# Two lanes in one load: keys by token and values, the source read as lane, token, row

## The reference

```python
scores = scale * np.matmul(q, k.transpose(0, 1, 3, 2))
gamma = 1.0 - 2.0 ** (-5.0 - np.arange(H, dtype=np.float32))
Dmat = np.where(rel >= 0, gamma[:, None, None] ** rel[None, :, :], 0.0)
attn = np.matmul(scores * Dmat[None], v)
x = attn.transpose(0, 2, 1, 3).reshape(B * S, H * D)          # 2304 x 512
xn = x / rms * rms_g
y = (silu(xn @ w_gate) * (xn @ w_val)) @ w_out                # 512 -> 1536 -> 512
g = where(h >= 1, h, where(h <= -1, 0, (h + 1) ** 2 / 4))     # h = y @ w_in, 512 -> 2048
out = g @ w_out2                                              # 2048 -> 512
```

## Time and profile before

| | |
|---|---|
| median of 3 runs | 922.66 us (922.09 to 923.28) |
| profiled execution | 925.14 us, its span 923.4 us |
| PE busy | 873.4 us, 95% |
| PEld busy | 829.0 us, 90% |
| DVE busy | 479.3 us, 52% |
| ACT busy | 434.7 us, 47% |
| POOL busy | 261.9 us, 28% |
| DMA | 124.26 MB, mean 135 GB/s |
| granted TensorE clock, mean | 0.985 |

### The profile page before, as it was taken

One profiled execution on the slowest core, in us unless ns is written; L12 is line 12 of the kernel. 1 busy time (PEld: TensorE's weight loads), 2 busy tenths in 40 slices (PEclk: granted clock), 3 DMA queues, 4 the chain that ended last, 5 costly groups with the idle time before them and its releaser, 6 DMA issues.

```text
span 923.4 us, 18183 instructions
## 1 busy us (share of the span) xinstructions
PE 873.4 (95%) x7712; PEld 829.0 (90%) x7712; DVE 479.3 (52%) x646; ACT 434.7 (47%) x704; POOL 261.9 (28%) x179
## 2 busy tenths in 40 slices
PE   4767799999999999999999998999999999999998
PEld 4666799999999999999999998999999888888886
DVE  3587975577875553522341668765656632222220
ACT  2545654445754554432131457877779732222110
POOL 0224764444954666000040321403134200000000
PEclk9897999999999999999999999999999999999999
DMA  6777133223234534533543134243439664433340
GB/s 202 218 219 229 37 111 97 98 97 98 93 103 147 183 98 150 184 104 103 182 147 128 53 129 149 103 136 116 141 117 299 211 166 129 114 114 114 114 119 29
DMA packets 124096, 124.26 MB, mean 135 GB/s; under 512 B 6256, under 2 KB 93424, under 8 KB 124016
## 3 DMA queue, kind: packets, MB, share of 16 engines
q1 hardware_dynamic: 124016, 123.11, 42.1%
HBM read 80.62 MB, written 42.47 MB: 133 GB/s over the span
## 4 chain that ended last, share of the span: by engine, by line
PE 78%; DVE 6%; DMA 5%; SPq 5%; ACT 3%; issue 2%; POOL 1%; DVEq 0%; ACTq 0%
PE pair L640 13%; PE pair L642 13%; PE pair L641 13%; PE pair L775 7%; PE pair L774 7%; PE pair L773 7%; PE pair L739 6%; PE pair L740 6%; PE pair L741 6%; DMA a_kt<-ktok 1%; DVE cb L1343 1%; SPq L346 1%; SPq L349 1%; DMA b_scratch<-cb 1%; ACT cl L911 1%
## 5 line engine op out<-in xcount | busy, mean ns | idle before, releaser
L640 PE MATMUL pair<-xc,wc 128*128 128x288 f32 x672 | 199.6, 297 | 0.9 <-ACT cp L898 0.6
L641 PE MATMUL pair<-xc,wc 128*128 128x288 f32 x672 | 198.3, 295 | 0.0
L642 PE MATMUL pair<-xc,wc 128*128 128x288 f32 x672 | 197.7, 294 | 0.0
L898 ACT ACTIVATE cp<-pair 128x576 f32<-128x576 f32 x160 | 103.3, 647 | 153.0 <-PE pair L642 146.7
L1431 POOL TENSOR_TENSOR wc<-wt,wc 128x512 fp32r<-128x512 f32 x84 | 123.0, 1488 | 94.6 <-ACT wc L831 67.9
L640 PE MATMUL pair<-xc,wr 128*128 128x288 f32 x448 | 133.9, 299 | 6.9 <-ACT cp L898 6.3
L641 PE MATMUL pair<-xc,wr 128*128 128x288 f32 x448 | 132.3, 295 | 0.0
L642 PE MATMUL pair<-xc,wr 128*128 128x288 f32 x448 | 131.8, 294 | 0.0
L640 PEld LDWEIGHTS pair<-xc,wc 128*128 128x128 f32 x672 | 126.0, 187 | 1.8 <-issue 1.5
L642 PEld LDWEIGHTS pair<-xc,wc 128*128 128x128 f32 x672 | 126.6, 188 | 0.0
L641 PEld LDWEIGHTS pair<-xc,wc 128*128 128x128 f32 x672 | 126.2, 188 | 0.0
(11 more groups left out here) (95 smaller groups left out, 1452.3 us busy)
## 6 DMA issues: line engine op xcount, KB each, us to landing
b_scratch<-cb SPq DMA_DIRECT2D x32, 576.0 KB, 2.9
bv_r<-b_scratch SPq DMA_DIRECT2D x18, 1024.0 KB, 5.8
a_scratch<-cb SPq DMA_DIRECT2D x24, 576.0 KB, 2.9
av_r<-a_scratch SPq DMA_DIRECT2D x8, 1728.0 KB, 8.5
wt<-wB SPq DMA_DIRECT2D x72, 128.0 KB, 2.9
a_k<-kT SPq DMA_DIRECT2D x16, 288.0 KB, 4.1
a_q<-qT SPq DMA_DIRECT2D x16, 288.0 KB, 4.6
y_scratch<-yo SPq DMA_DIRECT2D x8, 576.0 KB, 3.7
```

What stands on the lines that cost most here:

```text
L640: pe.matmul(o, wh, xh, start=FIRST[i] and j == 0, stop=False, skip_group_check=True)
L641: pe.matmul(o, wh, xl, start=False, stop=False, skip_group_check=True)
L642: mm = pe.matmul(o, wl, xh, start=False, stop=j == 1, skip_group_check=True)
L898: act.activation(copied(g, n)[:, :, :], pair[(X, Q, X, X)[n]][:, :, 0:HALF], ACT.Copy).then_inc(s_c, 1)
```

## The change

The two loads of the keys by token, one a lane, become one load that writes all 128 rows, and so do the two loads of the first four chunks of the values. The source is read as lane, token, row: first the 64 tokens of lane 0, each 512 floats, then the 64 tokens of lane 1. The ninth chunk of the values keeps its load. The waits count one load of a_kt and two of a_v a unit.

```diff
-                for l in range(2):
-                    rows, some = slice(C * l, C * l + C), slice(NL * l, NL * l + NL)
-                    sp.dma_start(a_kt[rows, i, :, :], ktok[b, p, :, some, :]).then_inc(d_kt[i], 16)
-                for l in range(2):
-                    rows, some = slice(C * l, C * l + C), slice(NL * l, NL * l + NL)
-                    sp.dma_start(a_v[rows, p, 0:NL, :], vtok[b, p, :, some, :]).then_inc(d_v[p], 16)
+                def lanes(src):
+                    return src.rearrange("t (l j) d -> l t (j d)", l=2)
+
+                sp.dma_start(a_kt[:, i, :, :].rearrange("s j d -> s (j d)"), lanes(ktok[b, p])).then_inc(d_kt[i], 16)
+                sp.dma_start(a_v[:, p, 0:NL, :].rearrange("s j d -> s (j d)"),
+                             lanes(vtok[b, p, :, 0:2 * NL, :])).then_inc(d_v[p], 16)
                 sp.dma_start(a_v[0:C, p, NL, :], vtok[b, p, :, NC - 1, :]).then_inc(d_v[p], 16)
@@ states
-                pe.wait_ge(d_v[p], 48 * (b + 1))
+                pe.wait_ge(d_v[p], 32 * (b + 1))
@@ decayed
-                act.wait_ge(d_kt[i], 32 * (u // NK + 1))
+                act.wait_ge(d_kt[i], 16 * (u // NK + 1))
```

## The result

The changed kernel takes 1034.6 us (median of 3 runs, 1033.78 to 1035.08), the kernel before 922.66 us: 1.121 times as long, 95% interval 1.119 to 1.124. Its profiled execution took 1035.08 us with a span of 1033.3, against 925.14 and 923.4: 109.9 us more.

The account below looks back on a forecast made before the run. Load issuing and moving were both taken as near their limits in the attention stage. Two engines needing 205.0 us for sixteen units start later stages 112.5 us later: 925.1 + 112.5 = 1037.6, put at 1035 us for timed runs; range 1005 to 1110.

Parts of the forecast that it names:

- Two engines: Attention stage: merged loads, divided along a source outermost axis of 2, run on two DMA engines; slower, chance 0.87.
- The rate: Attention stage: engines 0 and 1 each carry 301,056 bytes a unit at 23.5 GB/s, 12.8 us a unit, 205.0 us for sixteen.
- one rival: Attention stage: two engines at the stage's mean rate, 16.6 to 17.5 us a unit, 1096 to 1110 us; chance 0.17.
- The weight loads: Attention stage: eight weight loads of 128 KB, 64 KB an engine at 17.7 GB/s, add 3.7 us.
- Do the two engines run dry?: Attention stage: they stay fed, as three key buffers leave two whole units, 25 us of work, queued.
- The last values: End of the attention stage: last values land at 211.6 us, with completion about 212 us.
- From the last values to the first product: Attention stage's end: the last unit's states, copy and outputs, with gaps, take 4.7 us; L640 may start at 216.7.
- The 1.3 us given back: First products: POOL has its share of the first weight unit done, so a pause goes, 1 to 1.5 us.
- The signs: Profile: DMA share 0.15 to 0.2, 85 to 100 GB/s, L791 every 12 to 13 us, load waits over 100 us.
- TensorE's clock: Attention stage: TensorE may run at its lower clock level, hidden there; 1 or 2 us at the first product.
- Spread over all engines: Attention stage: merged loads as wide as any other, two issues a unit saved, about 915 us, between 906 and 923; chance 0.10.
- nothing won: Attention stage: loads use all engines, but the 1.2 us saved a unit turns into a longer hold, 923 us; chance 0.03.

Follow-up runs that it names:

- the four runs with 2 to 16 groups: Changed kernel, keys and values stored by the host so the merged loads' outermost source axis counts 2, 4, 8 or 16: 1034.2, 953.9, 926.6, 925.4 us.
- plain rows: Changed kernel, host storing each unit's keys and first eight value chunks as 128 back-to-back rows of 2 KB: 917.8 us, 0.992 to 0.996 times before.
- gaps: Changed kernel, merged loads reading 128 rows of 2 KB with 512 bytes unused behind each row: 918.3 us, 0.993 to 0.997 times before.
- three axes: Changed kernel, merged loads reading 16 blocks of 8 rows of 2 KB, 512 bytes unused behind each block: 925.4 us, 1.000 to 1.004 times before.

## Why the prediction was right

The forecast was 1035 us and the measured 1034.6. Part of this closeness is chance, as the steps show.

*Two engines.* Right, and it was the choice on which the sign hung. The trace of before could not show it. The packets (960 fewer, and two in flight at once for more than half of the stage), the share of 0.13 with 51 GB/s, and the four runs with 2 to 16 groups do.

*The rate.* Taken as 23.5 GB/s from one microsecond with all engines busy, 12.8 us a unit. Measured: 24.6 over a whole unit, 12.25 us; 25.5 in a stretch with almost only merged loads. So sixteen units were put 16 x 0.56 = 9 us too long. The means of 17 to 18 GB/s, which one rival rested on, belong to a stage in which all sixteen engines work; two engines left to themselves were faster, and that rival falls. The upper bound of 26.5 was nearer to such an engine than the stage's mean.

*The weight loads.* Expected 3.7 us in line on the same two engines; the step that holds them took 15.60 against 12.25, so 3.35 us.

*Do the two engines run dry?* No, as forecast, but not for the reason given. I let the three buffers of keys set how far the queue runs ahead, by two units or 25 us. The keys of the fourth unit were free to be issued from 19 us on, when the first unit's were decayed, and were issued at 34.21, as the queue was held behind the loads of the third unit until then; its lead is the 15 us seen above, and that was enough.

*The last values.* Expected to be there at 212 us. L559 of the last unit starts at 204.93 us: 7 us earlier, where the rate alone gives 9; the other 2 weren't traced.

*From the last values to the first product.* Sized too small. I took 4.7 us, as the sum of the last unit's own steps. The end of the stage after, which answers to the earlier trace rows:

```profile
204.93 1.13 PE L559 MATMUL pair<-a_v,a_kd 64*64 64x64 f32 x32 [6.93 <-issue]
...
206.12 0.22 ACT L798 ACTIVATE a_S<-pair 128x64 f32<-128x64 f32 x1 [3.49 <-PE pair L559]
206.44 2.18 DVE L1136 SCALAR_TENSOR_TENSOR a_S<-a_S,cdec_s,pair 128x64 f32<-128x64 f32 x7 [7.51 <-ACT a_S L798]
...
206.83 1.94 PE L583 MATMUL pair<-a_q,a_S 64*64 64x64 f32 x31
...
208.81 0.60 ACT L803 ACTIVATE xr<-pair 128x512 f32<-128x512 f32 x1 [2.46 <-PE pair L583]
...
209.66 0.92 PE L576 MATMUL pair<-a_r,a_v 64*64 64x64 f32 x36 [0.89 <-ACT xr L805]
...
210.37 1.10 PE L583 MATMUL pair<-a_q,a_S 64*64 64x64 f32 x32
...
211.40 0.40 PE L640 MATMUL pair<-xc,wc 128*128 128x288 f32 x1
```

The code has `states(15)`, `outputs(14)`, `outputs(15)` in a row. So the outputs of the unit before (1.94) and their way out of PSUM (0.60 and the small copy) stand before the last unit's own, and the stretch takes 6.5 us. The earlier trace rows could have said so: the same two instructions, L559 and the first L640, are 6.23 us apart there (96.64 to 102.87).

*The 1.3 us given back* at the first products didn't come: from the first L640 to the first copy L898 it was 5.84 us before and is 5.90 now. POOL's parts of the first weights are queued between the outputs' decays of units 14 and 15, so it does them in the last microseconds as before, however long it idled earlier.

Together: 7 us too late at the last values, 1.8 and 1.3 us too short behind them. The first product was forecast at 216.7 and came at 211.40; with the give-back that didn't come the shift is 108.5 us, not 112.5. Another 1.3 us appeared in the long rest (816.0 us from the first copy to the end, 814.7 before), whose cause wasn't looked for. The profiled execution is 109.9 us longer, the medians of the runs 111.9; the forecast of 112.5 came nearer to the latter than its working deserves.

*The signs.* Three of those named came true: 98 GB/s over the stage, a start of L791 every 11.7 to 12.8 us but for the step with the weights, and the rest of the kernel as before but shifted. The share is 0.30 and not 0.15 to 0.2: I had counted the fourteen other engines as almost idle, yet each carries 38 KB a unit at the slower pace of all sixteen. ScalarE's wait for keys is 85.3 us and not over 100. How long a merged load takes to land the trace doesn't give; the keys of the fourth unit reached ScalarE 15 us after their issue, most of it in line.

*TensorE's clock.* As supposed, it fell: a granted clock of 0.50, the level of 1.2 GHz, from 108 to 116 us with TensorE busy for 0.56 us of the eight, and 0.70 over the stage. It was hidden: L559 takes 317 ns where it took 265, in a stage that waits for loads.

*The rivals.* "Spread over all engines" has its price tested in three runs: 917.8 with plain rows, 918.3 with gaps, 925.4 with three axes, against a forecast of about 915 with 906 and 923 as its bounds; the third lies above them. (The bytes of a unit in it were added up wrongly: 288 + 288 + 512 + 32 are 1120 KB, 1.147 MB, not 1088; at 248 GB/s that is 4.6 us and not 4.5. The two engines' share of 256 + 38 KB was right, so the forecast doesn't hang on it.) The bound of the queue alone was out of reach, since the queue turned to waiting for TensorE. The rival "nothing won" had named just this, a hold in place of the issues, and in part it is what happened; "spread and faster" had named VectorE and POOL as late next, and not TensorE.

## What to carry to other kernels

Before two transfers are merged, write down the axes of both sides as the transfer will carry them and look at the outermost one: here a count of 2 put 256 KB on two engines of sixteen and cost 112 us of 923, where the same bytes with 128 rows outermost, laid out so by the host, save 5 us. The count of small packets, one for each load and engine, tells in one line how wide the loads of a kernel really are. And a saved issue is worth only what lies between it and the next wait: 19 us of queue time became 5, since the queue soon stood waiting for a buffer that TensorE held.

## What the runs showed of the hardware

Three things that I had not expected. Two DMA engines left almost to themselves move rows of 2 KB at 25.5 GB/s each (51 GB/s together), while in the stage of before, with all sixteen at work and packets of all sizes, a busy engine averages 18.1. It is not only the mix: by the packet records a packet of 2 KB takes 112 ns on average there and 89 in the changed kernel, with a median of 84 in both. So a busy share of 0.74 was not three quarters of what sixteen engines at 25.5 GB/s could move (214 of 408 GB/s is half). Second, behind loads that run on two engines SyncE's queue is held at each of the next two issues, mostly for about 5 us (128 KB an engine at 25.5 GB/s is 5.1), once it is some 15 us ahead of them. And five loads a unit cost 6 to 7 us more of the kernel's time when the source of the merged ones has three axes and not two, at the same width; their packets are slower (112 against 96 to 98 ns) and some issues longer (0.60 against 0.43 us), and what makes them so stays open.
